# First feed-forward layer in token chunks of 288, 384 and 480 in place of four of 288, with g kept in a ring and the buffers laid out anew

## The reference

```python
h = x @ w_in                                   # x: 1152 tokens x 512, w_in: 512 x 2048
neg, pos = h <= -1.0, h >= 1.0
g = np.where(pos, h, np.where(neg, 0.0, (h + 1.0) ** 2 / 4.0))
x2 = g @ w_out                                 # w_out: 2048 x 512
```

```python
logits = x2 @ w_gate                           # 1152 x 8
expert_idx = np.argmax(logits, axis=1)
y = np.maximum(disp[e] @ w1[e], 0.0) @ w2[e]   # disp[e]: the tokens of expert e
out[i] = gate_w[i] * y[expert_idx[i], pos[i]]
```

## Time and profile before

| | us |
|---|---|
| median of three runs | 310.76 (310.55 to 310.79) |
| profiled execution | 309.65 |
| its span | 307.8 |
| TensorE busy in the span | 300.6 |
| VectorE busy | 218.8 |
| ScalarE busy | 153.1 |
| GpSimd busy | 136.6 |

### The profile page before, as it was taken

The page is one execution under the profiler, slowest core; times in us unless marked ns, Lnnn a source line. Parts: engine busy times, 40 slices in busy tenths (PEclk is TensorE's granted clock), DMA queues, the critical chain, the costliest instruction groups (busy, mean ns, idle before and its releaser), DMA issues.

```text
span 307.8 us, 6950 instructions
## 1 busy us (share of the span) xinstructions
PE 300.6 (98%) x2667; PEld 247.3 (80%) x2667; DVE 218.8 (71%) x576; ACT 153.1 (50%) x337; POOL 136.6 (44%) x154
## 2 busy tenths in 40 slices
PE   7999999999999999999999999999999999999994
PEld 6666766666677988887999999898989899995563
DVE  5999998999977366997884567956775578852300
ACT  1786875867866144655551353446354546301130
POOL 4878997998997300564781002014011334010121
PEclk9999999999999999999999999999999999999998
DMA  8989899771447600000000409560024029079940
GB/s 163 160 195 226 213 178 181 194 187 36 154 105 181 215 0 2 0 2 2 0 2 4 75 0 352 204 107 3 2 47 70 0 85 425 38 242 375 404 160 9
DMA packets 75046, 38.47 MB, mean 125 GB/s; under 512 B 66008, under 2 KB 66016, under 8 KB 73988
## 3 DMA queue, kind: packets, MB, share of 16 engines
q1 hardware_dynamic: 72340, 36.74, 44.7%
q10 hardware_dynamic: 2416, 0.59, 1.0%
q0 software_dynamic: 256, 0.67, 0.7%
HBM read 32.66 MB, written 5.39 MB: 124 GB/s over the span
## 4 chain that ended last, share of the span: by engine, by line
PE 95%; DVE 2%; issue 1%; POOL 1%; ACT 0%; POOLq 0%; DVEq 0%
PE bank_a L1848 17%; PE bank_b L1848 17%; PE bank_out L1805 6%; PE bank_a L1706 4%; PE bank_b L1908 4%; PE bank_pt L1758 4%; PE bank_pt L1908 4%; PE bank_a L1782 3%; PE bank_b L1701 2%; PE bank_a L2087 2%; PE bank_out L1881 2%; PE bank_b L2087 2%; PE bank_out L1802 2%; PE bank_b L2097 2%; PE bank_out L2227 2%; PE bank_a L2097 2%
## 5 line engine op out<-in xcount | busy, mean ns | idle before, releaser
L723 POOL TENSOR_SCALAR prob<-prob,rl,gate_loc 128x512 f32<-128x512 f32 (+3 forms) x64 | 41.5, 664 | 10.6 <-DVE rl L1247 10.6
L1848 PE MATMUL bank_a<-x_hi,win_hi 128*128 128x288 f32 x128 | 39.3, 307 | 0.0
L1848 PE MATMUL bank_b<-x_hi,win_hi 128*128 128x288 f32 x128 | 38.2, 298 | 0.0
L1848 PE MATMUL bank_b<-x_lo,win_hi 128*128 128x288 f32 x128 | 38.0, 297 | 0.0
L1848 PE MATMUL bank_b<-x_hi,win_lo 128*128 128x288 f32 x128 | 38.0, 297 | 0.0
L1848 PE MATMUL bank_a<-x_hi,win_lo 128*128 128x288 f32 x128 | 38.0, 297 | 0.0
L1848 PE MATMUL bank_a<-x_lo,win_hi 128*128 128x288 f32 x128 | 38.0, 297 | 0.0
L974 ACT ACTIVATE g_raw<-bank_a,biases 128x576 f32<-128x576 f32 x16 | 11.9, 743 | 49.5 <-DVE sq L1324 49.5
L911 ACT ACTIVATE prob<-prob,negmax 128x512 f32<-128x512 f32 (+3 forms) x64 | 35.0, 548 | 0.3 <-DVE negmax L1197 0.3
L807 POOL TENSOR_TENSOR w_lo<-w_sb,w_hi 128x512 fp32r<-128x512 f32 x8 | 11.3, 1418 | 48.2 <-ACT w_hi L1017 48.2
L752 POOL TENSOR_TENSOR x_lo<-xT,x_hi 128x1152 fp32r<-128x1152 f32 x4 | 10.6, 2659 | 48.5 <-ACT x_hi L924 48.5
(11 more groups left out here) (334 smaller groups left out, 801.6 us busy)
## 6 DMA issues: line engine op xcount, KB each, us to landing
w_sb<-in_moe_w_dram SPq DMA_DIRECT2D x6, 2048.0 KB, 10.8
win_raw<-in_moe_w_in_dram SPq DMA_DIRECT2D x4, 1024.0 KB, 6.1
wout<-in_moe_w_out_dram SPq DMA_DIRECT2D x4, 1024.0 KB, 6.0
win_raw<-in_moe_w_in_dram SPq DMA_DIRECT2D x1, 4096.0 KB, 13.8
out_dram<-zero_row SPq DMA_DIRECT2D x8, 288.0 KB
x_d<-x_rows SPq DMA_DIRECT2D x32, 72.0 KB, 2.1
v_sb<-in_v_dram SPq DMA_DIRECT2D x16, 128.0 KB, 2.6
qn<-in_q_dram SPq DMA_DIRECT2D x24, 72.0 KB, 5.4
```

The source lines that it names most:

```text
L723: pool.tensor_scalar(prob[u][:, h, :], prob[u][:, h, :], rl[:, c:c + 1], gate_loc[:, 2 * j + h:2 * j + h + 1], ALU.mult, ALU.mult).then_in ...
L1848: last = pe.matmul(h_bank(d)[:, t, :], w[:, m, f:f + P], x[c % 2][:, m, :], start=(m == 0 and n == 0), stop=(m == KT - 1 and n == 2))
```

## The change

Nine tiles of 96 tokens remain behind chunk 0. In place of three chunks of three tiles they become one of four (384 tokens) and one of five (480). The chunks' inputs get buffers of their own (`x_hi[c]`, `x_lo[c]`), where before two pairs alternated; the 384-token chunk crosses from the first batch to the second, so its split is made in two pieces. All 16 feature tiles of g no longer fit at this width: g becomes a ring of eight tiles (`g_ring`, RING = 8), and a relu of step d >= 4 (in chunk 2 also of d = 0 and 2) waits until `logits` has read what stood in its slots. `logits` is moved so that it reads early. `wout` has three slots in place of four; w1 and w2 of the main expert stand apart, w2 in the ring's place, so its load waits for the last `logits` of chunk 2. ScalarE's and VectorE's splits of the expert's weights, GpSimd's, and the turns of x (four in each later chunk) are put in new places.

```diff
@@ -44,8 +44,14 @@
     SLOTS = slot_tiles * ST
     NTOK = N // ST
     CHUNK = 3 * ST
-    NCH = N // CHUNK
-    assert N % CHUNK == 0 and CHUNK <= 512
+    NR = slot_tiles
+    LATER = NTOK - NR
+    TILES = (NR, LATER // 2, LATER - LATER // 2)
+    NCH = len(TILES)
+    FROM = [sum(TILES[:c]) for c in range(NCH)]
+    NC = [ST * n for n in TILES]
+    NRM = max(TILES)
+    assert sum(TILES) == NTOK and N % ST == 0 and max(NC) <= 512
...
         ND = FT // 2
-        assert S == 2 * CHUNK and NR == slot_tiles
...
+        RING = 8
...
 
         def turns_of(c):
 
-            return ((), (0, 1), (2, 3, 4), (5, 6, 7))[c]
+            return ((), range(NPAIR // 2), range(NPAIR // 2, NPAIR))[c]
 
 
         def tiles_of(src, h):
@@ -617,9 +651,10 @@
             e0 = sp.value_load(first_e[0:1, 0:1], min_val=0, max_val=E - 1)
             sp.wait_ge(s_y, KT)
             first_weights(0, e0)
+            for j in turns_of(2):
+                store_rows(j)
+            sp.wait_ge(s_lq, NQ * (NCH - 1))
             second_weights(0, e0)
-            for j in range(turns_of(2)[0], NPAIR):
-                store_rows(j)
             sp.wait_ge(s_h, ND * NCH)
             sp.dma_start(win_raw[:, :, :], w_in.rearrange("(k p) f -> p k f", p=P)).then_inc(s_win, 16)
             sp.wait_ge(s_job, 1)
...
@@ -918,10 +976,12 @@
 
             def x_hi_part(c):
 
-                act.wait_ge(s_xe, KT if c < 2 else NPAIR)
-                if c > 1:
-                    act.wait_ge(s_h, ND * (c - 1))
-                act.activation(x_hi[c % 2][:, :, :], x_of(c), ACT.Copy).then_inc(s_xhi, 1)
+                act.wait_ge(s_xe, KT if c == 0 else NPAIR)
+                if c == 2:
+                    act.wait_ge(s_wp, NGROUP + 1)
+                for cols, x in x_pieces(c):
+                    last = act.activation(x_hi[c][:, :, cols], x, ACT.Copy)
+                last.then_inc(s_xhi, 1)
```

ScalarE, VectorE:

```diff
@@ -967,13 +1027,15 @@
                 act.wait_ge(s_c, g + 1)
                 if isinstance(c, int) and c == 0 and d == EARLY:
                     act.wait_ge(s_pv, NPAIR)
-                if isinstance(c, int) and c > 1 and d % 2 == 0:
-                    act.wait_ge(s_lq, NQ * (c - 2) + d // 2 + 1)
+                if isinstance(c, int) and c > 0 and d % 2 == 0:
+                    if d > 3:
+                        act.wait_ge(s_lq, NQ * (c - 1) + d // 2 - 1)
+                    elif c > 1:
+                        act.wait_ge(s_lq, NQ * (c - 1) + d // 2 - 1)
                 if isinstance(c, int) and c == 1 and d == 0:
                     act.wait_ge(s_y, KT)
-                act.activation(g_raw[:, 2 * d:2 * d + 2, :], h_bank(d), ACT.Relu, bias=biases[:, 1:2]).then_inc(s_re, 1)
-                act.activation(sq[d % 2][:, :, :], sq[d % 2][:, :, :], ACT.Square, scale=0.5,
-                               bias=biases[:, 0:1]).then_inc(s_sq, 1)
+                act.activation(g_of(c, d), h_bank(d, size(c)), ACT.Relu, bias=biases[:, 1:2]).then_inc(s_re, 1)
+                act.activation(sq_of(c, d), sq_of(c, d), ACT.Square, scale=0.5, bias=biases[:, 0:1]).then_inc(s_sq, 1)
...
-                    if c == 2 and d in (2, 3):
-                        first_hi(d - 2)
-                    if c == 3 and d < 2:
-                        first_hi(2 + d)
-                    if c == 3 and d in (3, 4):
-                        first_hi(1 + d)
-                    if c == 3 and d == 5:
+                    if c == 2 and d < 6:
+                        first_hi(d)
+                    if c == 2 and d == 6:
                         x2_hi_part()
...
-            second_hi(0)
...
-                if f < ET - 1:
-                    second_hi(f + 1)
+                if f > ET - 3:
+                    second_hi(f + 2 - ET)
+            for i in range(2, ET):
+                second_hi(i)
...
@@ -1321,13 +1381,12 @@
                 dve.wait_ge(s_h, ND * c + d + 1)
                 if not (isinstance(c, int) and c == 0 and d < 2):
                     dve.wait_ge(s_g, ND * c + d - 1)
-                dve.tensor_scalar(sq[d % 2][:, :, :], h_bank(d), -1.0, 1.0, ALU.max, ALU.min).then_inc(s_c, 1)
+                dve.tensor_scalar(sq_of(c, d), h_bank(d, size(c)), -1.0, 1.0, ALU.max, ALU.min).then_inc(s_c, 1)
 
             def add_terms(c, d):
 
-                two = slice(2 * d, 2 * d + 2)
                 dve.wait_ge(s_sq, ND * c + d + 1)
-                dve.tensor_tensor(g_raw[:, two, :], g_raw[:, two, :], sq[d % 2][:, :, :], ALU.add).then_inc(s_g, 1)
+                dve.tensor_tensor(g_of(c, d), g_of(c, d), sq_of(c, d), ALU.add).then_inc(s_g, 1)
...
@@ -1511,17 +1578,17 @@
                         clip(c, d)
                     if c > 0 and d < len(turns_of(c)):
                         turn_x(turns_of(c)[d])
-                    if c > 1 and d == 2:
-                        copy_lt(c)
                     if c > 0 and d == 4:
                         choose(c)
                     if c > 0 and d == 6:
                         place(c)
                     if d > 0:
                         add_terms(c, d - 1)
+                    if c > 1 and d == 1:
+                        copy_lt(c)
                     if c == 1 and d == 2:
                         dve.wait_ge(s_xl1, 1)
-                        dve.tensor_copy(lgT[:, :], bank_t[:, 0:CHUNK]).then_inc(s_xle, 1)
+                        dve.tensor_copy(lgT_of(1), bank_t[:, 0:CHUNK]).then_inc(s_xle, 1)
                     if c > 0 and d == 7:
                         gates_of(c)
                     if c > 0 and d == ND:
@@ -1561,10 +1628,8 @@
             hidden_lo(0)
             hidden_lo(1)
             copy_lt(NCH)
-            second_lo(0)
             hidden_lo(2)
             choose(NCH)
-            second_lo(1)
             hidden_lo(3)
             gates_of(NCH)
             place(NCH)
@@ -1572,7 +1637,9 @@
             hidden_lo(5)
             rank_tokens(NCH)
             hidden_lo(6)
+            second_lo(0)
             hidden_lo(7)
+            second_lo(1)
```

TensorE (`chunk` and `route_between`):

```diff
@@ -2028,15 +2098,13 @@
                     if first and d in (3, 5, 7):
                         gate_part((d - 3) // 2)
                     if c > 1 and d == 1:
-                        logits(c - 1, NQ - 2)
                         logits(c - 1, NQ - 1)
-                    if not first and d == ND - 3:
-                        logits(c, 0)
-                        logits(c, 1)
                     if c == 1 and d == 2:
                         first_logits()
                     if c > 0 and d == 3:
                         token_logits(c)
+                    if c > 0 and d in ((3, 4, 6) if c == 1 else (2, 4, 6)):
+                        logits(c, (d - 2) // 2)
                     if c > 0 and d == 5:
                         positions(c)
                     if c > 0 and d == 7:
@@ -2115,8 +2183,8 @@
 
             def route_between(f):
 
-                if f < 2:
-                    logits(NCH - 1, NQ - 2 + f)
+                if f == 1:
+                    logits(NCH - 1, NQ - 1)
                 if f == 2:
                     token_logits(NCH)
                 if f == 4:
```

More of the change, by code:

```diff
@@ new lines, in build_program @@
+        assert GSLOTS == 4 and FT * 32 == 512
+        W_SIZE = 4 * DT * F
+        assert W_SIZE == 4 * ET * DM and sq_at + W_SIZE <= w_turn_at and W_SIZE <= 4 * FT * CHUNK
+        assert 2 * W_SIZE <= g_at - xT_at and 2 * W_SIZE <= 4 * KT * DFF
+        w1_at = (sq_at, xT_at, win_lo_at)
+        w2_at = (g_at, xT_at + W_SIZE, win_lo_at + W_SIZE)
+        w1_sb = [sb(f"w1_sb{p}", [P, DT, F], F32, at=w1_at[p])[0] for p in range(OTHERS + 1)]
+        w2_sb = [sb(f"w2_sb{p}", [P, ET, DM], F32, at=w2_at[p])[0] for p in range(OTHERS + 1)]
@@ L1392, in choose, with tall, fields @@
+            def tall(ap, n):
+                return ap.unsqueeze(1).to_broadcast([ST, n, E])
+            def fields(c):
+                return (small[:, n, 0:TILES[c - 1]] for n in range(10))
             def choose(c):
+                mx, idx, pos, over, slot_f, total, total_e, handled, taken, pos2 = fields(c)
+                n = TILES[c - 1]
                 dve.wait_ge(s_lg, c)
-                step(c, "lg", dve.tensor_copy(lg[:, :, :], bank_o[0:ST, LG_AT:LG_AT + NR * E].rearrange("p (r e) -> p r e", e=E)))
+                step(c, "lg", dve.tensor_copy(lg[:, 0:n, :], bank_o[0:ST, LG_AT:LG_AT + n * E].rearrange("p (r e) -> p r e", e=E)))
@@ L1473, in place @@
                 after(c, "slotf")
-                step(c, "slot", dve.tensor_tensor(slot[:, c - 1, :], slot_f, over, ALU.add))
+                step(c, "slot", dve.tensor_tensor(slot[:, FROM[c - 1]:FROM[c - 1] + n], slot_f, over, ALU.add))
                 if c == 1:
@@ L1934, in token_logits @@
                     pe.wait_ge(s_r, step_no(c - 1, "listed"))
-                for r in range(NR):
-                    last = pe.matmul(bank_o[0:ST, LG_AT + r * E:LG_AT + (r + 1) * E], lgT[:, r * ST:(r + 1) * ST], sel[:, 0:E],
+                for r in range(TILES[c - 1]):
```

(17 more changed lines are left out.)

283 lines of the change are left out of this document (161 added, 122 removed).

## The result

| | us |
|---|---|
| before, median of 4 runs | 310.66 (310.55 to 310.79) |
| changed kernel, median of 4 runs | 337.93 (337.36 to 338.56) |
| ratio | 1.0883, 95% interval 1.0864 to 1.0901 |
| changed kernel, profiled execution | 337.36, span 335.6 |

What follows compares the result with a forecast made beforehand. TensorE, 98% busy, was taken as the bound, so any new wait is paid in full. -2.56 - 0.1 (logits calls) + 18.5 + 2.7 = +18.6, +24.8 with the clock, on 310.76: 335.6 us, range 328 to 342.

Steps and rivals of the forecast that it cites:

- five waits: Moved logits calls in chunks 1 and 2: TensorE waits for VectorE's clip, routing work and addition, 18.5 us together (17 to 20.5).
- clock: TensorE's clock falls in four of the five waits, each costing 1.55 us: 6.2 us (0 to 9.5).
- longer matmuls: First feed-forward layer, chunks 1 and 2: 192 fewer matmuls, each saving a fixed 13.3 ns: -2.56 us.
- end of chunk 2: Step into the main expert: waits of 1.6 (last logits), 0.6 (token logits), 0.5 (second_lo(0)); together 2.7 us (0.5 to 4.5).
- rival 1: Waits come in the later chunks but the clock stays: 329.4 us (327 to 331); chance 0.22.
- rival 4: Longer matmuls of the first layer save nothing, cost growing with columns: 338.2 us; chance 0.06.
- The load of w2: Main expert's 2 MB load behind chunk 2's third logits: lands after 7.8 us, wanted about 10 us after; costed at nothing.
- rival 3: w2 load lands 5 us late, so the expert's second layer waits about 3 us: 338.6 us; chance 0.06.
- three slots for w_out: In first_result, three slots in place of four: costed at nothing, up to 1 us if GpSimd's cover is gone.

Runs made afterwards that it cites:

- e1: Changed kernel with logits calls 0 to 2 of chunks 1 and 2 moved behind steps 3, 5 and 7: 310.65 us, ratio 1.0012.
- e2: Changed kernel with VectorE's addition of the step before put ahead of the clip at steps 2, 4, 6 of later chunks: 311.89 us, ratio 1.0062.
- e3: Kernel before, with its four chunks of 288, whole g, old buffers and loads; only logits moved as the change does: 342.66 us, ratio 1.1020.
- e4: Changed kernel with 20 unread matmuls of 288 columns ahead of each of the five waiting logits calls: 329.65 us, ratio 1.0604.
- e5: Separate kernel, not the reference's work: matmul steps at several widths, bursts with waits between; 131.9, 173.4, 216.6 ns at 288, 384, 480 columns; slowed burst 1.55 us more.
- e6: e1 with gates_of(2) ahead of the last clip and second_lo(0) ahead of hidden_lo(6): 311.42 us, ratio 1.0061.
- e7: e1 with the x2 split two steps earlier and second_lo(0) ahead of the last but one hidden_lo: 309.30 us, ratio 0.9951.

## Why the prediction was right, point by point

| term | forecast | in the trace of the changed kernel |
|---|---|---|
| five waits | 3.3, 4.1, 3.1, 3.75, 4.2: 18.5 | 3.21, 3.98, 2.98, 3.61, 4.05 idle: 17.8; by the forecast's count of starts 18.5 |
| clock | 4 falls, 6.2 | 5 falls, 8.8 |
| longer matmuls | -2.56 | -1.6 |
| end of chunk 2 | +2.7 | 1.40 + 0.26 + 0.41 idle: +2.1 |
| sum | +24.8 | +27.8 on the spans |

**The waits** are right in number, place and size. The forecast counts from the start of the last matmul: 189.60 - 186.06 = 3.54, less the 0.22 of an undisturbed step, is 3.32 where the terms add up to 3.34. The reason is also shown, not only the size: the calls one step later (e1), the additions ahead (e2) and the calls alone in the old kernel (e3) each give what the order says. That all of the pieces of this sum were in the trace of before, under no wait at all, is what made it exact: the distance from clip to addition did not matter there and was in the timeline nevertheless. (The rows give 1.18 ns an element for the longer clip, and the forecast went on with 1.1; its sums are 18.54 and 24.74 where it writes 18.6 and 24.8. Nothing hangs on either.)

**The clock** was right as a mechanism and 2.6 us too small. Steps behind a wait against 0.78 + 4.37 = 5.15 us at 384 columns, and against e4's 1.01 + 5.44 = 6.45 at 480: 6.78, 7.73, 7.99, 7.99 and 8.01, so 1.6, 2.6, 1.5, 1.5 and 1.6, together 8.8 us. All five waits took the clock along, not four, and one fall, the one that came ahead of TensorE's return to work, cost a microsecond more. The single price, 1.55 us, is what e5 measured. That it was hit is partly luck: the forecast took it from the start of the program as a rise of the clock, and the clock column of before shows none: it has 1.00 in that stretch (2.00 to 5.00), as it has ahead of TensorE's first instruction, so the slow first matmuls alone spoke for it. e4 took the 8.3 us back with the waits left in place, so rival 1 was wrong for the kernel as it is, and right for one whose TensorE is kept at work: its sum was 329.4, e4 has 329.65. How close that is, is luck again: the matmuls saved 1.0 us less than in that sum, and the end of chunk 2 cost 0.6 less. The Trainium skill ("TensorE: Matmul & The Clock Gate", section "What's actually happening") says that activity releases a clock that is otherwise throttled, and the dummy matmuls of e4 agree with it.

**Longer matmuls** were mis-sized by 1.0 us. 24 steps of 3.20 us were 76.8 us, and 8 of 4.16 and 8 of 5.24 are 75.2. At 384 columns the 13.3 ns held; at 480 there are 17 to 19. The forecast took the lower end as fixed by the only width in the trace. It had named the other end (nothing saved, rival 4), and the truth lies between.

**The end of chunk 2**: of the three waits worked out as 1.6, 0.6 and 0.5, there are 1.40, 0.26 and 0.41. The last hangs on the place of `second_lo(0)`, as the forecast had it: e6 and e7 put it ahead of one `hidden_lo`, and it is gone. The load of w2, costed at nothing, was free (rival 3 did not come: it landed 8.3 us after its issue, and the first piece was split in time), as were three slots for w_out.

The spans moved by 3.0 us more than forecast (the median came out 2.3 above it): the clock (+2.6) and the matmuls (+1.0), less 0.6 at the end.

**What the change was worth without the waits** is e1: nothing (1.0012). The 1.6 us from fewer matmuls are given back around the end of chunk 2: 1.2 + 0.6 + 0.4 us of waits. Of these 2.2 us nearly all hang on where GpSimd's subtraction and `second_lo(0)` stand, and not on the width: e7, with the same chunks, has 0.3 at the last logits and 0.3 before the token logits, and is 1.7 us faster than the kernel before, about what the matmuls save.

## What to carry to other kernels

When a consumer is moved earlier in an in-order list, look up on the producer's engine what stands between the instruction that it needs and the moment it could run: if the producer's own list has that instruction behind work which depends on the consumer's previous step, the consumer pays the whole chain. A wait on TensorE costs more than its length as soon as the clock falls with it, here about 1.5 us for each wait of 3 us or more and once 2.6, and this part can be bought back with matmuls that do nothing. At the end of the last chunk nothing hides VectorE's work, so a GpSimd operation that holds it up there is paid by TensorE: moving it, with one small split of VectorE's, brought about as much (e7 against e1) as the wider chunks save in matmuls.
